# The order of pair 0's and pair 1's attention products at the start of a retention and mixture-of-experts kernel

## What is computed

```python
state = np.zeros((B, H, D, D), dtype=np.float32)
for t in range(S):
    state = gamma[None, :, None, None] * state + np.einsum('bhd,bhe->bhde', k[:, :, t], v[:, :, t])
    y[:, :, t] = scale * np.einsum('bhd,bhde->bhe', q[:, :, t], state)
```

## Time and profile before

| | before |
|---|---|
| median of 3 runs | 421.69 us (421.29 to 423.27) |
| the profiled execution's own time | 421.05 us |
| its span, first to last instruction | 419.3 us |
| PE busy, share of the span | 406.3 us, 97% |
| DVE busy | 223.1 us, 53% |
| ACT busy | 196.5 us, 47% |
| POOL busy | 149.9 us, 36% |
| HBM read and written over the span | 58.49 MB and 10.22 MB, 164 GB/s |
| granted TensorE clock, mean | 0.994 |

### The profile page before, as it was taken

How to read it: one execution, slowest core, us unless ns; L and a number is a source line. 1 busy time by engine, 2 the same in 40 slices (tenths; PEclk the granted TensorE clock), 3 DMA queues, 4 the chain that set the end, 5 groups by cost and what they waited for, 6 DMA issues and landing times.

```text
span 419.3 us, 7163 instructions
## 1 busy us (share of the span) xinstructions
PE 406.3 (97%) x2601; PEld 343.2 (82%) x2602; DVE 223.1 (53%) x289; ACT 196.5 (47%) x276; POOL 149.9 (36%) x125
## 2 busy tenths in 40 slices
PE   7999999999999999999899999999999999999992
PEld 3888799887889987879688888888888888888871
DVE  4888749982004878577767312217641461725440
ACT  2334678670215765461618312228741462826450
POOL 3354872000000000027554612216872282653761
PEclk9999999999999999999999999999999999999997
DMA  8999900000520009551178571111569108356100
GB/s 294 407 411 416 384 2 2 0 2 0 200 101 0 2 0 368 234 202 63 48 307 363 166 332 50 25 50 39 222 270 402 50 25 341 123 221 262 37 26 15
DMA packets 16153, 67.75 MB, mean 162 GB/s; under 512 B 2623, under 2 KB 4159, under 8 KB 11776
## 3 DMA queue, kind: packets, MB, share of 16 engines
q1 hardware_dynamic: 12928, 58.87, 35.4%
q0 software_dynamic: 2912, 8.13, 5.8%
q10 hardware_dynamic: 288, 0.41, 0.3%
HBM read 58.49 MB, written 10.22 MB: 164 GB/s over the span
## 4 chain that ended last, share of the span: by engine, by line
PE 90%; DMA 6%; ACT 1%; DVE 1%; issue 1%; POOL 0%; ACTq 0%; SPq 0%; POOLq 0%; DVEq 0%
PE ps L971 25%; PE ps L973 25%; PE ps L972 25%; DMA kv<-qkv 4%; PE ps L1261 3%; PE ps L1211 2%; PE ps L1022 2%; PE ps L1019 2%; PE ps L1001 2%; PE ps L1068 1%; PE ps L985 1%; DMA xg<-x_rows,gnow 1%; ACT kv L544 1%; PE ps L1047 0%; DMA x_rows<-x2n 0%
## 5 line engine op out<-in xcount | busy, mean ns | idle before, releaser
L427 POOL TENSOR_TENSOR wx<-raw_w,wx 128x1024 fp32r<-128x1024 f32 x21 | 53.6, 2567 | 14.7 <-ACT wx L583 14.6
L971 PE MATMUL ps<-wx,xT 128*128 128x512 f32 x136 | 54.5, 401 | 1.6 <-DVE xT L900 1.3
L583 ACT CAST wx<-raw_w 128x1024 fp32r<-128x1024 f32 x56 | 54.8, 1058 | 1.9 <-issue 1.3
L971 PE MATMUL ps<-wx,hT 128*128 128x512 f32 x136 | 54.5, 401 | 0.2 <-DVE hT L908 0.2
L973 PE MATMUL ps<-wx,hT 128*128 128x512 f32 x136 | 53.2, 391 | 0.0
L973 PE MATMUL ps<-wx,xT 128*128 128x512 f32 x136 | 53.1, 391 | 0.0
L972 PE MATMUL ps<-wx,hT 128*128 128x512 f32 x136 | 53.1, 390 | 0.0
L972 PE MATMUL ps<-wx,xT 128*128 128x512 f32 x136 | 53.0, 390 | 0.0
L891 DVE TENSOR_TENSOR wx<-raw_w,wx 128x1024 fp32r<-128x1024 f32 x35 | 48.1, 1421 | 4.8 <-ACT wx L583 4.8
L645 ACT CAST hT<-ps 128x512 fp32r<-128x512 f32 x34 | 18.3, 591 | 57.2 <-PE ps L1261 57.2
L971 PE MATMUL ps<-x,win 128*128 128x384 f32 x128 | 43.2, 337 | 0.0
(11 more groups left out here) (163 smaller groups left out, 800.8 us busy)
## 6 DMA issues: line engine op xcount, KB each, us to landing
raw_w<-w_exp SPq DMA_DIRECT2D x28, 1024.0 KB, 8.9
qk<-qkv SPq DMA_DIRECT2D x7, 768.0 KB, 9.8
raw_first<-w_exp SPq DMA_DIRECT2D x4, 1024.0 KB, 7.7
kv<-qkv SPq DMA_DIRECT2D x4, 768.0 KB, 11.5
x_rows<-x2n SPq DMA_DIRECT2D x11, 256.0 KB, 2.8
kv<-qkv SPq DMA_DIRECT2D x7, 384.0 KB, 9.9
x_early<-x2n SPq DMA_DIRECT2D x10, 256.0 KB, 2.3
win_raw<-w_in SPq DMA_DIRECT2D x4, 512.0 KB, 12.3
```

The costliest lines, as they stand in the source:

```text
L427: ins = nc.gpsimd.tensor_tensor(wx[:, slot, 1, c], raw, wx[:, slot, 0, c].bitcast(F32), ALU.subtract)
L583: nc.scalar.copy(wx[:, slot, 0, c], raw).then_inc(wx_hi[w], 1)
L971: mm(o, lh, rl, start=first, stop=False)
```

## The change

In `values`, groups n = 0 and n = 2 (the first values of pairs 0 and 1) first issue all three within-chunk blocks, only then wait for the scaled q and for the state, and then issue the two state's blocks. The first block opens the bank for accumulation and the others do not. In the order by hand, the two idle matmuls behind scores(0, 1) are gone, and updates(1) moves from behind scores(1, 0) to behind values(0, 1). Later pairs keep their order.

```diff
             def values(i, g):
                 j, n = i % 4, 2 * i + g
                 y = psY[n % 3]
-                if g == 0:
+                within_first = n in (0, 2)
+                if g == 0 and not within_first:
                     pe.wait_ge(q_scaled, i + 1)
                 if n >= 3:
                     pe.wait_ge(ylo_done, n - 2)
                 pe.wait_ge(masked, n + 1)
-                for k in range(GC):
+
+                def within(k, first, last):
                     c = GC * g + k
...
+                if within_first:
+                    for k in range(GC):
+                        within(k, k == 0, k == 0)
+                    pe.wait_ge(q_scaled, i + 1)
+                    for k in range(1, GC):
+                        last = before(k, False, True)
+                else:
+                    for k in range(GC):
+                        c = GC * g + k
+                        if c:
+                            before(k, True, False)
+                        last = within(k, c == 0, True)
                 last.then_inc(pv_done, 1)
 
             scores(0, 0)
             warm_up(6, psY[2])
             updates(0)
             scores(0, 1)
-            warm_up(2, psY[2])
             pe.wait_ge(zeroed, 2)
             for i in range(B * NP_):
                 values(i, 0)
                 if i + 1 < B * NP_:
                     scores(i + 1, 0)
-                    updates(i + 1)
+                    if i:
+                        updates(i + 1)
                 values(i, 1)
+                if i == 0:
+                    updates(1)
                 if i + 1 < B * NP_:
                     scores(i + 1, 1)
```

More of the change, by code:

```diff
@@ L1012, in values, with before @@
                 pe.wait_ge(masked, n + 1)
-                for k in range(GC):
+                def within(k, first, last):
                     c = GC * g + k
-                    cs, ys = slice(P * c, P * c + P), slice(P * k, P * k + P)
+                    for h in range(2):
+                        ins = mm(y[D * h:D * h + D, P * k:P * k + P], kv[j][:, 1, P * c + D * h:P * c + D * h + D],
+                                 probs[g][:, h, k, :], start=first, stop=last, skip_group_check=True)
+                    return ins
+                def before(k, first, last):
+                    c = GC * g + k
                     if c == 1:
                         pe.wait_ge(st_done, 2 * i + 2)
-                    for h in range(2 if c else 0):
-                        mm(y[D * h:D * h + D, ys], state[i % 2][:, h, :, c - 1], qs[j][:, cs], start=True,
-                           stop=False, skip_group_check=True)
                     for h in range(2):
-                        last = mm(y[D * h:D * h + D, ys], kv[j][:, 1, P * c + D * h:P * c + D * h + D],
-                                  probs[g][:, h, k, :], start=(c == 0), stop=True, skip_group_check=True)
+                        ins = mm(y[D * h:D * h + D, P * k:P * k + P], state[i % 2][:, h, :, c - 1],
+                                 qs[j][:, P * c:P * c + P], start=first, stop=last, skip_group_check=True)
+                    return ins
+                if within_first:
[6 more added lines that the diff above has]
+                    for k in range(GC):
+                        c = GC * g + k
+                        if c:
+                            before(k, True, False)
+                        last = within(k, c == 0, True)
                 last.then_inc(pv_done, 1)
```

## The result

| | before | after |
|---|---|---|
| median of 22 executions | 421.95 us (421.14 to 423.27) | 423.1 us (421.56 to 424.72) |
| ratio to before, 95% interval | | 1.0026 (1.0015 to 1.0037) |
| the profiled execution, its span | 421.05, 419.3 us | 422.26, 420.2 us |
| granted TensorE clock, mean | 0.994 | 0.995 |

The changed kernel is **slower by 0.26%**, 1.15 us between the medians. The prediction said no change, 421.7, with a range up to 422.9, so the measured median lies outside its range.

What follows compares the result with a forecast made beforehand. TensorE is 97% busy, but updates(6) at 38.33 starts from pair 6's kv load on a full queue. The 0.44 us gain is given back within one pair: sum 0.00 us, forecast 421.7, range 420.8 to 422.9.

Steps and rivals of the forecast that it cites:

- the attention part: First 49 us: 0.44 us gained at pair 0, given back within one pair; updates(6) at 38.33 in both kernels.
- Sum: 0.00 us: Whole kernel: no net change against the profiled 421.05 us; chance 0.78 that nothing of the gain is left at 38.33.
- the disturbed loads: Rival: pair 4's loads, issued 1.07 us earlier, take traffic from pair 3's; up to +0.87 us, 422.6; chance 0.05.
- The 0.20 before updates(6): TensorE stood 0.20 us waiting for pair 6's load, so it may come up to 0.20 us later without cost.
- the step that cost the shorter stream at nothing: Two idle matmuls behind scores(0, 1) vanish; no instruction is added to any queue; their removal by itself moves nothing.
- the 0.31 us hold at 15.90: In values(1, 0), TensorE stands 0.31 us from 15.90 until scan(1)'s state is usable at 16.21, a new wait.
- the clock rival: Fewer idle matmuls and a new hold at 15.90 lower TensorE's clock for 3.2 us: +1.4 us, 423.1; chance 0.03.

Runs made afterwards that it cites:

- after_third: The changed kernel timed a third time, no further edit; median 423.30 us, ratio to the kernel before 1.0022.
- hold: The changed kernel with pair 4's loads held until the first values of pair 1 are finished; median 422.03 us, ratio to the kernel before 1.0007.
- shift4: The kernel before with two idle matmuls fewer behind scores(0, 0), old order kept; median 421.75 us, ratio 1.0009.
- undo_move: The changed kernel with updates(1) back in its old place; median 422.48 us, ratio to the kernel before 1.0017.
- pad_again: Second run of the changed kernel with two more idle matmuls behind scores(0, 0), about the old stream length; median 422.13 us, ratio to the kernel before 1.0003.
- pad: The changed kernel with two more idle matmuls behind scores(0, 0), about the old stream length; median 421.57 us, ratio to the kernel before 1.0002.
- before_handoff: The kernel before with four idle matmuls added right ahead of the expert loop; 421.98 us, ratio 0.9997.
- shift2: The kernel before with one idle matmul fewer behind scores(0, 0); median 421.84 us, ratio 1.0001.
- long4: The kernel before with two idle matmuls more behind scores(0, 0); median 422.01 us, ratio 1.0005.

## Why the prediction was wrong

**Right, within 0.2 us: the attention part.** The within-chunk records ran in the hold, scores(1, 0) came 3.32 us behind updates(0) (11.50 - 8.18) against a forecast 3.22 and 3.66 before, a gain of 0.34 (0.44 was forecast). Updates(1) came 5.62 behind it, forecast 5.58. The state of pair 1 was used 8.23 behind it, forecast 8.15, and its hold exists. Scores(2, 0) is within 0.1 of the forecast. Updates(6) still hangs on a load in the first trace; in the six other traces of the new order it follows updates(5) by 5.10 to 5.11 us, TensorE's own pace, and no load holds it. "Sum: 0.00 us" stands for this part within 0.2, and so do the spans of the executions without the fall.

**Right in kind, without weight: the disturbed loads.** Priced as a rival at up to +0.87. The mechanism is there, but it hit pair 2's k and not pair 3's. The 1.2 us of slack that this k had took most of it. The 0.20 before updates(6), which the prediction counted on as cover, took little: in after_third TensorE waits 0.38 us at updates(2), and updates(6) is then 30.63 behind updates(0), the latest of all. About 0.2 us between the medians is left.

**Wrong: the step that cost the shorter stream at nothing.** The prediction says that no instruction is added to any queue and ends its sum at updates(6). It counted the two idle matmuls only by the time they take and the activity they give where they stand. It didn't count them as instructions in the stream of TensorE, whose number decides what happens 190 us later: with two fewer, in either order, one packet of code comes later, the matmuls stand once for 1.65 to 1.81 us ahead of the expert loop, and in 34 of 82 executions the clock falls behind it, for 1.6 us. With the old number there was none. The falls make 1.0 of the 1.15 us between the medians; the rest isn't clear of the scatter.

**Right in kind, wrong in place, chance and weight: the clock.** The rival had the clock fall behind the 0.31 us hold at 15.90, for +1.4 us, with a chance of 0.03. The price was nearly right: 1.6 was measured, and the fallen stretch (3.4 us, 208.98 to 212.40 in after_third) is about as long as the one at the kernel's start from which I took it. The granted clock that read 1.00 there was no evidence: the trace's clock record begins at 4.82 us, and the view counts what lies ahead of it as 1.00. The place was wrong. At 15.90 nothing fell; the clock fell at 209 us, behind a hold of 1.8 us that I never looked at, since it lay outside the part that the change touches. The argument against the rival, that 1.36 us of standing cost nothing, was sound for the place it looked at: the three falls that were caught lie behind holds of 1.81 us, and holds up to 1.46 brought none in seven traces. It said nothing about a longer hold elsewhere.

Last, the width. With the fall in about half of the executions the median depends on which half is larger: 422.13, 423.1 and 423.30 in three sets of the same changed kernel. A range reaching to the clock rival's 423.1 would just have held the result.

**What stays open.** Which way the late fetch leads to the earlier end of the gather isn't shown; that the code packet holds up some of the gathered rows on a DMA engine fits the fourteen traces, but nothing was run on it. Nor is it shown why TensorE, with xT ready earlier, starts no sooner: in the changed kernel's first trace the hold ends 1.17 us behind the end of the low part of xT, before 0.79, and the profile names nothing it waited for. That it waits for the loop's code is likely, and untested. And nothing was run on why the same kernel has the fall in only half of its executions. The traces' clock records say more than the text so far, though. Full clock is first on record at 4.12, 4.18 and 4.99 us in the three traces with a fall (hold, after_third, shift4), and the fall comes at 208.92, 208.98 and 209.79, in each 204.80 us later. In the four traces of the short stream without a fall it is first on record at 5.78 to 6.64 us, though one of them, undo_move, has the same hold of 1.81. An early start alone isn't enough either: pad_again has 4.34 and the kernel before 4.82, with their shorter holds and no fall. So which executions fall seems to be settled by when the clock rose near the start, beside the hold; seven traces fit this, and no run tests it.

## What to carry to other kernels

Removing idle or useful instructions anywhere ahead of a loop shifts that engine's code, so compare the holds of the whole trace, not only of the part that was edited, and test a small regression with a kernel that restores only the length. Where a hold of TensorE ahead of dense work grows beyond those that it ran through before, look at the span and mean clock of every execution, not only at the profiled one; a few idle matmuls in that hold took the fall away here and cost nothing that could be measured. And a gain at the head of a stage is soon gone when the work that it leads to waits for something else: here for the scan, and with the move undone for a load.

## What the runs showed of the hardware that was not expected

- Four instructions or so fewer in TensorE's stream (two idle matmuls, each with its weight load) took the packet of code near the gather from 202 to 204 us to behind 204 us, and with it both holds of TensorE changed. Two fewer instructions (one idle matmul) did nothing.
- The fall comes in part of the executions only: 34 long executions in the 82 of the four kernels with the shorter stream and nothing in the hold (changed 23 of 46, hold 4, shift4 4, undo_move 3 of 12 each), none in the 187 with a stream at most one idle matmul shorter than before's (116 + 11 of the kernel before, 60 of pad, pad_again, before_handoff, shift2 and long4). Three of the four kernels were caught in one by the profile, each with its clock at 1.2 GHz for 3.4 us, and with the fall 204.80 us behind the first record of full clock; the other counts rest on span and mean clock.
- The step of the expert loop is 12.25 us in some traces and 12.29 in others of the same kernel, 0.65 us over 16 steps. It was 12.29 in six of seven traces with the shorter stream and in one of seven others; no run shows why.
- A load issued 0.8 us earlier on a full queue pushed the landing of one issued 8.6 us before it (5.38 against 14.01) back by 1.1 us or more.
